# Attention stage: three VectorE operations with a scalar operand written as operations on two tensors

## The reference, cut to what matters

```python
scores = scale * np.matmul(x, state.transpose(0, 1, 3, 2))
scores = scores - scores.max(-1, keepdims=True)
a = np.exp(scores)
a /= a.sum(-1, keepdims=True) + 1e-09
xread = np.matmul(a, state)
scores2 = scale * np.matmul(state, x.transpose(0, 1, 3, 2))
scores2 = scores2 - scores2.max(-1, keepdims=True)
a2 = np.exp(scores2)
a2 /= a2.sum(-1, keepdims=True) + 1e-09
sread = np.matmul(a2, x)
```

## Time and profile before

| | |
|---|---|
| median of 3 runs | 1362.72 us (1361.45 to 1363.45) |
| the profiled execution: its own time | 1367.19 us |
| its span, first to last instruction | 1365.4 us |
| mean granted TensorE clock | 0.991 |
| busy: PE, DVE, ACT, POOL | 1339.8, 843.3, 425.0, 166.2 us |
| chain that ended last | PE 90%, DVE 6%, issue 1%, DMA 1%, ACT 1% |

### The profile page before, as it was taken

How to read it: one execution, slowest core, us unless ns; L and a number is a source line. 1 busy time by engine, 2 the same in 40 slices (tenths; PEclk the granted TensorE clock), 3 DMA queues, 4 the chain that set the end, 5 groups by cost and what they waited for, 6 DMA issues and landing times.

```text
span 1365.4 us, 22360 instructions
## 1 busy us (share of the span) xinstructions
PE 1339.8 (98%) x7818; PEld 1155.7 (85%) x7819; DVE 843.3 (62%) x1108; ACT 425.0 (31%) x611; POOL 166.2 (12%) x228
## 2 busy tenths in 40 slices
PE   8999899999989999998999999999999999999998
PEld 7888688888878888887999999999978888888887
DVE  6899752226474444438667777678866666666652
ACT  6887431113343232325111221013322222222211
POOL 3564112121222122221000000000000000000000
PEclk9999899999999999998999999999999999999999
DMA  8884371115465425335334333434444444444453
GB/s 272 281 289 157 118 248 42 42 39 177 142 220 207 169 69 230 100 108 185 135 133 146 123 128 125 147 131 145 143 116 116 116 115 115 115 115 116 122 117 53
DMA packets 180258, 193.41 MB, mean 142 GB/s; under 512 B 24832, under 2 KB 130304, under 8 KB 179712
## 3 DMA queue, kind: packets, MB, share of 16 engines
q1 hardware_dynamic: 172960, 172.41, 40.2%
q0 software_dynamic: 6112, 19.93, 4.2%
q10 hardware_dynamic: 1152, 0.66, 0.2%
HBM read 125.07 MB, written 67.37 MB: 141 GB/s over the span
## 4 chain that ended last, share of the span: by engine, by line
PE 90%; DVE 6%; issue 1%; DMA 1%; ACT 1%; DVEq 0%; POOL 0%; ACTq 0%; SPq 0%; POOLq 0%
PE ps_p L403 13%; PE ps_p L405 13%; PE ps_p L404 13%; PE ps_h L403 5%; PE ps_h L405 5%; PE ps_h L404 5%; PE ps_y L403 5%; PE ps_o L404 5%; PE ps_o L405 5%; PE ps_y L405 5%; PE ps_o L403 5%; PE ps_y L404 5%; PE ps_hT L1651 2%; PE ps_xT L1645 1%; DVE a L1084 1%; PE ps_sr L1535 1%
## 5 line engine op out<-in xcount | busy, mean ns | idle before, releaser
L403 PE MATMUL ps_p<-b_hi,w_hi 128*128 128x272 f32 x896 | 259.5, 290 | 3.9 <-DVE b_lo L1369 3.9
L405 PE MATMUL ps_p<-b_hi,w_lo 128*128 128x272 f32 x896 | 259.5, 290 | 0.0
L404 PE MATMUL ps_p<-b_lo,w_hi 128*128 128x272 f32 x896 | 259.5, 290 | 0.0
L403 PEld LDWEIGHTS ps_p<-b_hi,w_hi 128*128 128x128 f32 x896 | 169.5, 189 | 4.9 <-DVE b_lo L1369 4.9
L405 PEld LDWEIGHTS ps_p<-b_hi,w_lo 128*128 128x128 f32 x896 | 169.8, 190 | 0.0
L404 PEld LDWEIGHTS ps_p<-b_lo,w_hi 128*128 128x128 f32 x896 | 169.3, 189 | 0.0
L1307 DVE COPY hid<-ps_h 128x512 f32<-128x512 f32 x72 | 49.8, 692 | 168.7 <-PE ps_h L405 164.6
L403 PE MATMUL ps_h<-w_hi,xgT_hi 128*128 128x512 f32 x296 | 121.7, 411 | 2.0 <-DVE xgT_lo L1178 2.0
L403 PE MATMUL ps_y<-w_hi,hidT_hi 128*128 128x512 f32 x296 | 123.5, 417 | 0.0
L1436 DVE SCALAR_TENSOR_TENSOR neg<-gt,alpha 128x2048 f32<-128x2048 f32 x33 | 75.6, 2292 | 71.6 <-DMA gt<-acts 71.6
L1447 DVE TENSOR_TENSOR g_lo<-gt,g_hi 128x2048 fp32r<-128x2048 f32 x34 | 77.9, 2292 | 65.5 <-ACT g_hi L975 65.5
(11 more groups left out here) (259 smaller groups left out, 2349.2 us busy)
## 6 DMA issues: line engine op xcount, KB each, us to landing
acts<-gb SPq DMA_DIRECT2D x128, 272.0 KB, 2.1
stage<-in_moe_w SPq DMA_DIRECT2D x32, 1024.0 KB, 5.4
gt<-acts SPq DMA_DIRECT2D x32, 1024.0 KB, 6.1
xN_all<-in_xN SPq DMA_DIRECT2D x8, 1024.0 KB, 6.2
rows_x<-xrow SPq DMA_DIRECT2D x32, 256.0 KB, 2.6
out_rows<-orow SPq DMA_DIRECT2D x32, 256.0 KB, 2.0
yz<-rows_y SPq DMA_DIRECT2D x30, 256.0 KB
xs_all<-in_xT SPq DMA_DIRECT2D x7, 1024.0 KB, 6.7
```

The lines of the kernel that those rows point to most:

```text
L403: pe.matmul(out, s_hi, m_hi, start=start, stop=False)
L404: pe.matmul(out, s_hi, m_lo, start=False, stop=False)
L405: return pe.matmul(out, s_lo, m_hi, start=False, stop=stop)
```

## The change

A constant tile `eps` of one column with 1e-9 is added and filled by GpSimd at the start, so `const_ready` counts to 13 and 15 instead of 12 and 14. The additions of 1e-9 to `csum` (128x2) and to `rsum` (128x32) become `tensor_tensor` with `eps` broadcast, and the multiplication of `a2` with `cinv` becomes `tensor_tensor` with the column of `cinv` broadcast over the 512 columns. No instruction changes its place on any engine; GpSimd has one more (the fill of `eps`).

```diff
+        eps = sb("eps", [P, 1], c=ab)
...
+            pool.memset(eps[:], 1e-9).then_inc(const_ready, 1)
...
-            pool.wait_ge(const_ready, 12)
+            pool.wait_ge(const_ready, 13)
...
-                    dve.tensor_scalar(csume[:], csum[:], 1e-9, None, ALU.add).then_inc(s2_eps, 1)
+                    dve.tensor_tensor(csume[:], csum[:], eps[:].to_broadcast([P, 2]), ALU.add).then_inc(s2_eps, 1)
...
                     for g in range(2):
-                        dve.tensor_scalar(a2[par][:, g, :], a2[par][:, g, :], cinv[:, g:g + 1], None, ALU.mult)\
+                        dve.tensor_tensor(a2[par][:, g, :], a2[par][:, g, :], cinv[:, g:g + 1].to_broadcast([P, S]), ALU.mult)\
                            .then_inc(a2_ready, 1)
...
-                    dve.tensor_scalar(rmax[:], rsum[:], 1e-9, None, ALU.add).then_inc(s1_eps, 1)
+                    dve.tensor_tensor(rmax[:], rsum[:], eps[:].to_broadcast([P, SC * H]), ALU.add).then_inc(s1_eps, 1)
...
-            pe.wait_ge(const_ready, 14)
+            pe.wait_ge(const_ready, 15)
```

More of the change, by code:

```diff
@@ L651, in _ @@
                                pattern=[[1, P]], channel_multiplier=-1).then_inc(const_ready, 1)
-            pool.wait_ge(const_ready, 14)
+            pool.wait_ge(const_ready, 15)
             pool.dma_start(rows_x[0:1, :], zrow).then_inc(zero_stored, 16)
@@ L1109, in turn @@
                     copy_srow(b, early)
-            dve.wait_ge(const_ready, 14)
+            dve.wait_ge(const_ready, 15)
             dve.tensor_copy(iota_p[:], iota_i[:]).then_inc(const_cast, 1)
```

## The result

The changed kernel takes 1367.87 us (median of 20 runs), the kernel before 1364.12 us in 20 runs (the three of the section on the time before are the first of them): ratio 1.0028, 95% interval 1.0020 to 1.0036, so 3.8 us slower (2.7 to 4.9).

The account below looks back on a forecast made before the run. TensorE was taken as the bound, its attention transposes waiting for the multiplications. The terms 2.76 + 0.42 + 0.05 + 0.1 + 0.06 = 3.4 us took 1362.72 to 1366.1 us; range 1360.5 to 1368.0.

Parts of the forecast that it names:

- the question: In the attention, whether a tensor_tensor is held by GpSimd as well; the trace was read as yes.
- Plain cost: Multiplications of a2 with nothing in the way: 693 against 483 ns, +0.21 us each, +0.42 a pair.
- Held cost: Multiplications of a2 that wait for GpSimd: +0.23 us each, +0.46 a turn, bounds 0.42 and 0.54.
- Turns 1 to 6 pay in full: PE's transposes already wait for the multiplications there, so nothing covers the addition: 6 x 0.46 = 2.76 us.
- Additions 0.1: Additions of 1e-9 to csum and rsum as tensor_tensor: together 0.1 us, bounds 0 and 0.25.
- fill 0.06: Fill of eps at the start, ahead of PE's first product: 0.06 us, bounds 0 and 0.12.
- turn 7 0.05: In the last attention turn DVE waits 0.37 us for PE, so of 0.42 us only 0.05 stays.
- The first rival: Multiplications with a broadcast column don't wait for GpSimd: 2.3 us less, 1360.4 us; chance 11%.
- The second rival: VectorE's second multiplication goes ahead of GpSimd's rounding: +1.1 us with fill and additions, 1363.8, no change; chance 10%.
- The third rival: Between attention and 200 us, 1 to 3 us of the 3.4 vanish by gather waits or clock: 1363 to 1365; 16%.

Follow-up runs that it names:

- e5: Changed kernel with column sums plus constant (again added by a scalar) and their reciprocals in PSUM, so each multiplication has one SBUF input: 1362.83 us, ratio 0.9988.
- e2: Changed kernel with the multiplications of a2 by a scalar again, leaving only the additions and the new tile: 1364.17 us, ratio 1.0003.
- e1: Kernel before with only the 16 multiplications of a2 written as tensor_tensor: 1366.69 us, ratio 1.0019 to the kernel before.
- e4: Changed kernel with GpSimd's rounding of half a weight chunk moved ahead of its two xs_lo in each turn: 1363.51 us, ratio 0.9995.
- e6: Changed kernel with the two multiplications of a2 written as one tensor_tensor of 128x1024: 1364.19 us, ratio 1.0002.
- e3: Kernel before with GpSimd's rounding of half a weight chunk moved ahead of its two xs_lo in each turn: 1363.02 us, ratio 0.9991.

## Why the prediction was right

The time, the sign and the mechanism held: 1366.1 us against 1362.72 is +3.4 us, measured +3.8 (2.7 to 4.9). The time itself, 1367.87 us, is 1.8 us above the forecast and only 0.1 under the end of the range, 1368.0: the 20 runs of the kernel before have a median 1.4 us above that of the three from which the forecast started. That it stayed in the range owes something to luck, and so does the size of the difference, as the parts show.

- *A `tensor_tensor` with both inputs in SBUF is held too* (the question, read from L1023, L1015 and L1102): shown in the profile after for the multiplications and the addition, and by its opposite in e5.
- *Plain cost, +0.21 us each*: 0.689 against 0.483, right. From turn 0 to turn 1 the distance grew from 12.11 to 12.51 us, 0.40 where 0.42 was forecast.
- *Held cost, chosen +0.23 each between 0.21 and 0.27*: measured 0.55 - 0.29 = 0.26 each, the upper value, the one from the single row L1023. The caution about a single row cost accuracy.
- *Turns 1 to 6 pay in full*: this step failed for turn 1. TensorE's products there end at 35.03 us in the kernel before and L1084 ends at 34.50, so the turn had cover; the distance from turn 1 to turn 2 stayed (31.20 to 45.91 before, 30.83 to 45.55 after, 14.7 both). The list of waits had counted six, and I took them for turns 1 to 6 without looking at each; they are turns 0 and 2 to 6. Turns 2 to 6 paid more than 0.46 each: from 45.91 to 121.26 is 75.35 us, from 45.55 to 123.41 it is 77.86, so 2.5 us in five turns, 0.50 each, which is what TensorE's waits there grew by (2.0 to 4.5). The two errors nearly cancel, and that is luck: 2.5 against 2.76 forecast for turns 1 to 6.
- *Additions 0.1, fill 0.06, turn 7 0.05*: 0.0 in the distance of e2, 0.03, and 0.1 from turn 7 to the gather (18.83 us before, 18.90 after). The parts that the traces show sum to 0.4 + 2.5 + 0.1 + 0.03 = 3.0 us. That the runs show 3.8 is within their interval. The executions of one kernel come at several mean granted clocks, from 0.991 (the longest) to 0.995, and a median moves with how many fall on each. Against the 35 runs of the kernel before that stand beside e1 to e4, the changed kernel's mean is 2.8 us longer at 0.995 (1365.0, 5 runs, against 1362.2, 12 runs), 3.3 at 0.991 (1369.8, 5 runs, against 1366.5, 9 runs) and 3.7 at 0.992 (7 and 3 runs). So a part of the 0.8 may be this mix; those 35 runs may be of another chip, the 20 runs beside the changed kernel have no clock on record, and whether the rest is real stays open.
- *The first rival's price*: e5 made its case true. The multiplications were free, and the gain was not 2.7 us but 1.3 from turn 1 to turn 7 (90.06 to 88.78 us). Two things were wrong in the price. Of the 2.7 us of waits 0.64 stand in turn 0, where the longer form only adds, so 2.0 could be won; and TensorE gave part of that back in its own products. With the 0.4 us that turn 0 loses, that is 0.9 us less than before by the traces and 1.6 (0.1 to 3.3) by the runs, where the rival was priced at 2.3.
- *The second rival* (VectorE's next instruction goes ahead of GpSimd's): it never did; the second multiplication was held by the rounding in each of turns 2, 3 and 5, and by moving the rounding (e4) or joining the two (e6) its effect, one wait less, was made by hand.
- *The third rival* (lost on the way): nothing of it shows: the gather comes 3.0 us later, and the medians differ by 3.8.

## What to carry to other kernels

When a small instruction has a long duration, compare it with the same one at a quiet moment: the difference is a wait inside the instruction that stands in no list of its engine's waits. Here a held instruction of 512 columns ended 0.29 us (by a scalar) or 0.55 us (two tensors) behind GpSimd's. Changing a form of operation does not help if the new form needs the same thing; ask where each input and the output lies, and count how often in a turn the operation has to wait. Before pricing waits, look up in which turns they stand: one of the six here was not where it was taken to be. And look at what the waiting engine does next: of the 2.0 us of waits in turns 2 to 6, removing them gained 1.6 us in e3 and 1.3 in e5.

## What the runs showed of the hardware

- VectorE operations of 128x2 wait for GpSimd's instruction as large ones do: 0.15 us alone, 2.6 us behind `xs_lo`, with a scalar or with a tensor.
- The same `tensor_tensor` over 128x512 takes 0.69 us alone and up to 3.19 us beside GpSimd with its second input in SBUF, and 0.68 us always with it in PSUM; a `tensor_scalar` that writes PSUM is not held either (0.164 us in all 8 turns). The section Who interferes with whom of the Trainium skill's "SBUF — State Buffer" says this of operations with at most one input in SBUF outside the fast modes, and these rows agree.
- Held, the `tensor_tensor` ends 0.14 us sooner than wait plus its length alone (0.55 behind GpSimd for 0.69, 1.09 for 1.23), and the `tensor_scalar` 0.19 us sooner (0.29 for 0.48).
